# High parts one bank ahead of the low parts in the second product, and exchanged banks for half tiles

## The chip, the cores and the metric

The kernel runs on one core of a Trainium2 chip. The metric is the device time of one execution in microseconds. The unchanged kernel took 1166.94 us, the median of three runs (1163.73, 1166.94 and 1168.14).

## What is computed

Three stages over 7168 tokens of width 192, in float32:

- an attention-like convolution: for each token and each of 8 heads, a softmax over 7 taps weights the token and its 6 predecessors;
- a mixture of 8 experts in which each token goes to its best two, chosen by noisy logits;
- a second mixture of 8 experts in which each token goes to its best one.

An expert is two products with a ReLU between them. This is the part that matters here:

```python
h = np.maximum(x[mask] @ w1[e], 0.0)      # 192 -> 1024
out[mask] += top2_w[mask, k, None] * (h @ w2[e])   # 1024 -> 192
```

The second mixture is the same with one choice: `ye = h @ w2[e]`, times the gate's probability.

## The kernel before

**Numbers in two parts.** Matmuls run on fp32r operands, and each operand is split: a high part, which ScalarE rounds off, and a low part, which is the rest and which VectorE works out. The products high x high, high x low and low x high are added up in PSUM.

**Passes and tiles.** The first mixture is done in two passes (p = 0 and 1, one for each half of the tokens), the second in two more (p = 2 and 3). In each pass the tokens are sorted by expert into tiles of 256 rows (`T`); where at most 128 rows are left over for an expert, its last tile is a half tile of 128. Every engine has its own instruction stream and its own loop over the tiles, and they meet at semaphores. `g0 + j` is a tile's number over all passes.

**One full tile on TensorE** (`tile`, L1866): `up` (L1780) makes h, the product with w1, as 8 chunks `f` of 128 columns of w1 by 256 tokens, two chunks to each of the four banks of `ps_h` (banks 0 and 1 from chunks 0 to 3, banks 2 and 3 from chunks 4 to 7). Each chunk takes four matmuls (L1787, L1788, L1791, L1794); the first that needs xa_lo, the low part of the tile's rows, is L1791. Banks 0 and 1 are signalled after `up_low` (L1771), banks 2 and 3 at the end. Then `down` (L1839), the product with w2: for each of 8 chunks of h and each of the tile's two halves `u`, one matmul of the high part of h with both parts of w2 (L1849, 400 columns in the first two passes, 384 in the others) and one of the low part of h with the high part of w2 (L1850, 200 or 192 columns). Every fourth such matmul pair begins a bank, and there TensorE waits for the low part of that bank (L1843). After six pairs it turns the next tile's rows (`next_rows`, L1823): four transposes (L1764, L1765) of rows that GpSimd gathered by an indirect DMA (L584).

**ScalarE** (`tile`, L1476): `copy_high` (L1465) reads a bank of `ps_h` through the ReLU into `h_hi` (L1468), twice; then a middle part `mid_tile` (L1445) with side work and the next expert's w1a, after which it releases `ps_x`; then `copy_high` twice more; then the high parts of the next tile's rows (`split_rows`, L1395: xa_hi, L1397, and xb_hh, L1400, with the list for the next gather, L1504, between them); then it reads the low half of y (L1519 or L1525).

**VectorE** (`tile`, L1055): some side work (`before_splits`; in the first pass products of the convolution, L933), then four low parts `h_lo` (L1060), one a bank, each after that bank's `h_hi_ready`; then `after_splits` (sums of the convolution, L943), pieces of the next expert's weights (w1a L990, w1b L998), xa_lo and xb_lo of the next tile (L1042, L1043), w2 (L1013), and y of this tile (L1077 or L1080), which TensorE must have seen before its next `down`.

**A half tile.** `up_half` (L1803) makes h the other way round, 128 tokens by 512 columns, in banks 0 and 1 ("unturned rows"). ScalarE copies them out through the ReLU (`copy_rows`, L1471), TensorE turns them into banks 2 and 3 (L1819), and ScalarE reads those with `copy_high` into the second half of `h_hi`. The third read stands before ScalarE's middle part, the fourth behind it. VectorE runs all four low parts (L1060) in the order of the banks also here; the first two are of the unturned rows and nobody uses them. `down_half` (L1853) waits for the third low part before its first matmul (L1862) and for the fourth before its fifth pair; the next rows are turned after three pairs. `side` (L1746), work of TensorE for the routing of later passes, stands at the end of `up_half`.

## Time and profile before

| What | Value |
|---|---|
| Median of the runs | 1166.94 us (1163.73 to 1168.14) |
| The profiled execution's own time | 1160.52 us |
| Its span, first to last instruction | 1158.8 us |
| TensorE: matmuls busy | 1076.2 us, 93% |
| TensorE: weight loads busy | 1006.7 us, 87% |
| VectorE busy | 797.4 us, 69% |
| ScalarE busy | 561.2 us, 48% |
| GpSimd busy | 483.4 us, 42% |
| Mean granted TensorE clock | 0.977 |

The busy time of an engine is the sum over its instructions; matmuls are pipelined and their ends are modelled, so starts tell more than durations. In the rows further below an instruction is given by its start, its duration, its engine and line, what it writes and reads, and in brackets how long its engine stood idle before it and whose end released it.

### The profile page before, as it was taken

What the parts mean: (1) busy time and instruction counts of PE and PEld (TensorE: products, weight loads), DVE (VectorE), ACT (ScalarE), POOL (GpSimd) and SP (SyncE); (2) the same over time, 40 slices, a digit from 0 to 9 for tenths busy, and PEclk for the clock granted to TensorE, in tenths of its full rate; (3) what the DMA queues carried; (4) which work ended last, traced back from release to release, by engine and by line L of the source; (5) the groups of instructions that cost most, each with busy time, mean ns of one, the idle gap of its engine ahead of it and who ended that gap; (6) DMA issues with size and microseconds to landing.
All of it is one profiled execution on the core that took longest, in us unless ns stands there. A gap on an engine that the chain in (4) does not pass through costs nothing.

```text
span 1158.8 us, 29428 instructions
## 1 busy us (share of the span) xinstructions
PE 1076.2 (93%) x7894; PEld 1006.7 (87%) x7895; DVE 797.4 (69%) x1432; ACT 561.2 (48%) x1236; POOL 483.4 (42%) x527
## 2 busy tenths in 40 slices
PE   4998799889999999999999899999998898999995
PEld 3778699889999899999999899898988898898895
DVE  8998899998478655456656765556767765656652
ACT  3345335444634444455555344436665554555542
POOL 1000355555355444444444344444444543444442
PEclk9998899999999999999999999999999999999998
DMA  8449132342332233455544333337854643543510
GB/s 261 114 125 268 55 106 86 101 130 73 96 112 75 90 89 99 120 159 167 153 149 144 87 76 98 104 91 232 241 165 123 164 112 100 149 126 106 150 42 23
DMA packets 105109, 143.75 MB, mean 124 GB/s; under 512 B 27818, under 2 KB 82413, under 8 KB 104812
## 3 DMA queue, kind: packets, MB, share of 16 engines
q1 hardware_dynamic: 85612, 99.74, 29.8%
q0 software_dynamic: 19456, 43.53, 13.0%
q8 instruction: 17, 0.28, 0.1%
q14 instruction: 24, 0.20, 0.1%
HBM read 111.53 MB, written 35.09 MB: 127 GB/s over the span
## 4 chain that ended last, share of the span: by engine, by line
PE 75%; DVE 8%; DMA 6%; issue 6%; ACT 2%; DVEq 1%; POOL 1%; ACTq 0%; POOLq 0%; SPq 0%
PE ps_y L1849 20%; PE ps_y L1850 9%; PE ps_h L1787 7%; PE ps_h L1791 6%; PE ps_h L1788 6%; PE ps_h L1794 6%; DMA row<-x_rows,read_now 5%; PE ps_h L1775 4%; PE ps_h L1619 3%; PE ps_y L1862 2%; PE ps_x L1764 2%; PE ps_x L1765 2%; DVE h_lo L1060 2%; DMA w_more<-in_moe_w_dram 1%; PE ps_y L1863 1%
## 5 line engine op out<-in xcount | busy, mean ns | idle before, releaser
L1849 PE MATMUL ps_y<-w_hl,h_hi 128*128 128x400 f32 (+1 forms) x1344 | 411.5, 368 | 9.3 <-DVE h_lo L1060 7.6
L1060 DVE SCALAR_TENSOR_TENSOR h_lo<-ps_h,h_hi 128x512 fp32r<-128x512 f32 x404 | 259.4, 685 | 161.9 <-ACT h_hi L1468 129.0
L584 POOL DMA_INDIRECT row<-x_rows,read_now x200 | 225.3, 1127 | 303.9 <-ACT read_now L1504 259.1
L1850 PE MATMUL ps_y<-w_hl,h_lo 128*128 128x200 f32 (+1 forms) x1344 | 341.4, 254 | 0.0
L1468 ACT ACTIVATE h_hi<-ps_h 128x512 fp32r<-128x512 f32 x370 | 202.7, 595 | 222.7 <-PE ps_h L1775 137.7
L1849 PEld LDWEIGHTS ps_y<-w_hl,h_hi 128*128 128x128 f32 x1344 | 253.3, 189 | 13.2 <-DVE h_lo L1060 10.2
L1850 PEld LDWEIGHTS ps_y<-w_hl,h_lo 128*128 128x128 f32 x1344 | 257.5, 192 | 0.0
L1787 PE MATMUL ps_h<-xa_hi,w1a_hi 128*128 128x256 f32 x672 | 201.9, 300 | 3.1 <-ACT xa_hi L1397 2.5
L1791 PE MATMUL ps_h<-xa_lo,w1a_hi 128*128 128x256 f32 x672 | 190.5, 284 | 2.1 <-DVE xa_lo L1042 1.2
L1788 PE MATMUL ps_h<-xa_hi,w1a_lo 128*128 128x256 f32 x672 | 189.2, 282 | 0.0
L1794 PE MATMUL ps_h<-xb_hh,w1b_hl 128*128 128x256 f32 x672 | 188.6, 281 | 0.0
L602 POOL DMA_INDIRECT y_rows<-y,write_now x128 | 135.3, 1057 | 78.9 <-POOL write_now L597 58.5
L1787 PEld LDWEIGHTS ps_h<-xa_hi,w1a_hi 128*128 128x128 f32 x672 | 126.5, 188 | 15.8 <-ACT xa_hi L1397 3.0
L1791 PEld LDWEIGHTS ps_h<-xa_lo,w1a_hi 128*128 128x128 f32 x672 | 126.6, 188 | 3.1 <-DVE xa_lo L1042 1.8
L1788 PEld LDWEIGHTS ps_h<-xa_hi,w1a_lo 128*128 128x128 f32 x672 | 127.1, 189 | 0.0
L1794 PEld LDWEIGHTS ps_h<-xb_hh,w1b_hl 128*128 128x128 f32 x672 | 126.8, 189 | 0.0
L1397 ACT ACTIVATE xa_hi<-ps_x 128x256 fp32r<-128x256 f32 x101 | 38.8, 385 | 121.5 <-PE ps_x L1765 114.6
L602 POOL DMA_INDIRECT out_dram<-y,write_now x74 | 78.1, 1056 | 45.4 <-POOL write_now L597 33.2
L1042 DVE TENSOR_TENSOR xa_lo<-ps_x,xa_hi 128x256 fp32r<-128x256 f32 x101 | 42.4, 420 | 56.9 <-ACT xb_hh L1400 56.4
L1519 ACT ACTIVATE y_lo<-ps_y 128x400 f32<-128x400 f32 x64 | 32.3, 504 | 99.5 <-PE ps_y L1850 91.1
L597 POOL COPY write_now<-write_to 128x2 int32 x101 | 37.3, 369 | 103.1 <-DVE y L1077 52.0
L1077 DVE TENSOR_TENSOR y<-ps_y,y_lo 128x400 f32<-128x400 f32 x64 | 36.6, 572 | 46.0 <-ACT y_lo L1519 39.6
(245 smaller groups left out, 1665.1 us busy)
## 6 DMA issues: line engine op xcount, KB each, us to landing
w_raw<-in_moe_w_dram SPq DMA_DIRECT2D x32, 768.0 KB
w1a_raw<-in_moe_w_dram SPq DMA_DIRECT2D x32, 512.0 KB
w1b_raw<-in_moe_w_dram SPq DMA_DIRECT2D x64, 256.0 KB
x_rows<-tok SPq DMA_DIRECT2D x14, 512.0 KB, 3.3
x_rows<-tok SPq DMA_DIRECT2D x28, 256.0 KB
x_pad<-in_x_dram SPq DMA_DIRECT2D x2, 2688.0 KB, 11.7
row<-x_rows,read_now POOLq DMA_INDIRECT x200
x_pad<-y_rows SPq DMA_DIRECT2D x14, 200.0 KB
```

What stands on the lines that cost most here:

```text
L584: pool.indirect_dma_start(out=row[:, u, 0:XW if p < C else SCALED_W], out_offset=None, in_=x_rows[p], in_offset=bass.IndirectOffsetOnAxis( ...
L602: pool.indirect_dma_start(out=dst, out_offset=bass.IndirectOffsetOnAxis(ap=write_now[:, u:u + 1], axis=0), in_=y[:, u, 0:width], in_offset ...
L1042: nc.vector.tensor_tensor(xa_lo[:, :], ps_x[:, 0, :], xa_hi[:, :].bitcast(F32), ALU.subtract).then_inc(x_lo_ready, 1)
L1060: nc.vector.scalar_tensor_tensor(out=h_lo[:, i * GF:(i + 1) * GF, :], in0=ps_h[:, i, :].rearrange("p (f t) -> p f t", f=GF), scalar=0.0, i ...
L1468: act.activation(h_hi[:, i * GF:(i + 1) * GF, :], ps_h[:, i, :].rearrange("p (f t) -> p f t", f=GF), ACT.Relu).then_inc(h_hi_ready, 1)
L1775: last = nc.tensor.matmul(up_bank(f), w1b_hl[b][half, f * P:(f + 1) * P], xb_lo[half, :], start=(f // 2 == FC // 4), stop=(FC // 2 - 2 <= ...
L1787: nc.tensor.matmul(dst[f % 2], w1a_hi[b][:, cols], xa_hi[:, :], start=(f0 == 0), stop=False)
L1788: nc.tensor.matmul(dst[f % 2], w1a_lo[b][:, cols], xa_hi[:, :], start=False, stop=False)
L1791: nc.tensor.matmul(dst[f % 2], w1a_hi[b][:, cols], xa_lo[:, :], start=False, stop=False)
L1794: last = nc.tensor.matmul(dst[f % 2], w1b_hl[b][:, cols], xb_hh[:, :], start=False, stop=(f >= FC - 2))
L1849: nc.tensor.matmul(first, h_hi[:, i, cols], both_w, start=(i == 0), stop=False)
L1850: last = nc.tensor.matmul(second, h_lo[:, i, cols], high_w, start=False, stop=(i == FC - 1))
```

## The change

In full tiles, `down` runs over five steps k. Step k does the four high matmuls of bank k (k below 4) and, alternating with them, the four low matmuls of bank k - 1 (k above 0). High matmuls wait for `h_hi_ready`, low ones for `h_lo_ready`. The next rows are turned at the start of step 2.

In half tiles, the unturned rows are made in banks 2 and 3 and turned into banks 0 and 1, and the turned parts go to the first half of `h_hi`. ScalarE's copies of unturned rows have a semaphore of their own, `rows_copied`; the second turned bank signals three banks at once, so that VectorE's low parts of banks 2 and 3 (of rows that nobody uses) come last. `down_half` has three steps in the manner of `down`. `side` and the turning of the next rows stand after its first four high matmuls.

Since VectorE may still be reading banks 2 and 3 when the product is over, `up` waits for all of the tile before's low parts ahead of its fifth chunk, and `up_half` ahead of its first.

```diff
--- before.py
+++ after.py
@@ -249,7 +249,7 @@
         y_loaded = [sem(f"y_loaded{c}") for c in range(C)]
         scales_copied = sem("scales_copied")
         scales_seen = sem("scales_seen")
-        rows_seen = sem("rows_seen")
+        rows_copied = sem("rows_copied")
         w1a_loaded = sem("w1a_loaded")
         w1b_loaded = sem("w1b_loaded")
         w2_loaded = sem("w2_loaded")
@@ -1184,6 +1184,7 @@
             for p in (1, 2):
                 dve.sem_inc(columns_done[p + 1], FIRST[p])
             dve.sem_inc(y_ready, 1)
+            dve.sem_inc(h_lo_ready, NG)
             nc.vector.memset(h_hi[:, :, :].bitcast(F32), 0.0).then_inc(zeros_made, 1)
             for w in gate_w_b:
                 nc.vector.memset(w[0:DR, 1, :], 0.0).then_inc(consts_made, 1)
@@ -1471,7 +1472,13 @@
             def copy_rows(g0, j, i):
 
                 act.wait_ge(h_ps, (g0 + j) * NG + (i + 1))
-                act.activation(h_rows[i], ps_h[:, i, :], ACT.Relu).then_inc(h_hi_ready, 1)
+                act.activation(h_rows[i], ps_h[:, NG // 2 + i, :], ACT.Relu).then_inc(rows_copied, 1)
+
+            def copy_turned(g0, j, i, signals=1):
+
+                act.wait_ge(h_ps, (g0 + j) * NG + (NG // 2 + i + 1))
+                act.activation(h_hi[:, i * GF:(i + 1) * GF, :], ps_h[:, i, :].rearrange("p (f t) -> p f t", f=GF),
+                               ACT.Copy).then_inc(h_hi_ready, signals)
 
             def tile(p, g0, n, b0, full, j, e, ahead):
 
@@ -1483,11 +1490,14 @@
                 with act.Else():
                     for i in range(NG // 2):
                         copy_rows(g0, j, i)
-                    copy_high(g0, j, NG // 2)
+                    copy_turned(g0, j, 0)
                 mid_tile(p, j, b0, ahead)
                 with act.If(j < full):
-                    copy_high(g0, j, NG // 2)
-                copy_high(g0, j, NG // 2 + 1)
+                    for i in range(NG // 2, NG):
+                        copy_high(g0, j, i)
+                    act.sem_inc(rows_copied, 2)
+                with act.Else():
+                    copy_turned(g0, j, 1, 1 + NG // 2)
                 if ahead is not None:
                     with act.If(j == b0):
                         split_w1b(*ahead)
@@ -1777,9 +1787,15 @@
                     if f == FC // 2 - 1:
                         last.then_inc(h_ps, 2)
 
+            def lows(g, k):
+
+                return (g + 1) * NG + k
+
             def up(p, g0, j, b):
 
                 for f0 in range(0, FC, 2):
+                    if f0 == FC // 2:
+                        pe.wait_ge(h_lo_ready, lows(g0 + j, 0))
                     pair = (f0, f0 + 1)
                     dst = [up_bank(f) for f in pair]
                     for f in pair:
@@ -1803,7 +1819,9 @@
             def up_half(p, g0, j, b):
 
                 for i in range(NG // 2):
-                    dst = ps_h[:, i, :]
+                    dst = ps_h[:, NG // 2 + i, :]
+                    if i == 0:
+                        pe.wait_ge(h_lo_ready, lows(g0 + j, 0))
                     cols = slice(i * 512, (i + 1) * 512)
                     nc.tensor.matmul(dst, xa_hi[:, 0:P], w1a_hi[b][:, cols], start=True, stop=False)
                     nc.tensor.matmul(dst, xa_hi[:, 0:P], w1a_lo[b][:, cols], start=False, stop=False)
@@ -1814,11 +1832,10 @@
                     pe.wait_ge(x_lo_ready, 2 * (g0 + j) + 2)
                     nc.tensor.matmul(dst, xb_lo[:, 0:P], w1b_hl[b][:, cols], start=False, stop=True).then_inc(h_ps, 1)
                 for i in range(NG // 2):
-                    pe.wait_ge(h_hi_ready, (g0 + j) * NG + (i + 1))
+                    pe.wait_ge(rows_copied, (g0 + j) * 2 + (i + 1))
                     for q in range(FC // 2):
-                        last = nc.tensor.transpose(ps_h[:, NG // 2 + i, q * P:(q + 1) * P], h_rows[i][:, q * P:(q + 1) * P], ident[:, :])
+                        last = nc.tensor.transpose(ps_h[:, i, q * P:(q + 1) * P], h_rows[i][:, q * P:(q + 1) * P], ident[:, :])
                     last.then_inc(h_ps, 1)
-                side(p, j)
 
             def next_rows(p, g0, n, j):
 
@@ -1838,29 +1855,52 @@
 
             def down(p, g0, n, b, j):
 
-                for i, f in enumerate(sorted(range(FC), key=place_of)):
-                    if i % GF == 0:
-                        pe.wait_ge(h_lo_ready, (g0 + j) * NG + (i // GF + 1))
-                    if i == FC // 4 + 1:
+                order = sorted(range(FC), key=place_of)
+                for k in range(NG + 1):
+                    if k == 2:
                         next_rows(p, g0, n, j)
-                    for u in range(SUB):
+                    if k < NG:
+                        pe.wait_ge(h_hi_ready, (g0 + j) * NG + (k + 1))
+                    for m in range(GF * SUB):
+                        u = m % SUB
                         cols = slice(u * P, (u + 1) * P)
-                        first, second, both_w, high_w = down_operands(p, b, f, u)
-                        nc.tensor.matmul(first, h_hi[:, i, cols], both_w, start=(i == 0), stop=False)
-                        last = nc.tensor.matmul(second, h_lo[:, i, cols], high_w, start=False, stop=(i == FC - 1))
+                        if k < NG:
+                            i = k * GF + m // SUB
+                            first, _, both_w, _ = down_operands(p, b, order[i], u)
+                            nc.tensor.matmul(first, h_hi[:, i, cols], both_w, start=(i == 0), stop=False)
+                        if k > 0:
+                            i = (k - 1) * GF + m // SUB
+                            if m == 0:
+                                pe.wait_ge(h_lo_ready, lows(g0 + j, k))
+                            _, second, _, high_w = down_operands(p, b, order[i], u)
+                            last = nc.tensor.matmul(second, h_lo[:, i, cols], high_w, start=False, stop=(i == FC - 1))
                 last.then_inc(y_ps, 1)
 
+            def half_at(f):
+                return f // 2
+
+            def half_cols(f):
+                return slice(f % 2 * P, f % 2 * P + P)
+
             def down_half(p, g0, n, b, j):
 
-                for f in range(FC):
-                    if f % 4 == 0:
-                        pe.wait_ge(h_lo_ready, (g0 + j) * NG + (NG // 2 + f // 4 + 1))
-                    if f == FC // 2 - 1:
+                for k in range(3):
+                    if k == 1:
+                        side(p, j)
                         next_rows(p, g0, n, j)
-                    at, cols = FC // 2 + f // 2, slice(f % 2 * P, f % 2 * P + P)
-                    first, second, both_w, high_w = down_operands(p, b, f, 0)
-                    nc.tensor.matmul(first, h_hi[:, at, cols], both_w, start=(f == 0), stop=False)
-                    last = nc.tensor.matmul(second, h_lo[:, at, cols], high_w, start=False, stop=(f == FC - 1))
+                    if k < 2:
+                        pe.wait_ge(h_hi_ready, (g0 + j) * NG + (k + 1))
+                    for m in range(FC // 2):
+                        if k < 2:
+                            f = k * (FC // 2) + m
+                            first, _, both_w, _ = down_operands(p, b, f, 0)
+                            nc.tensor.matmul(first, h_hi[:, half_at(f), half_cols(f)], both_w, start=(f == 0), stop=False)
+                        if k > 0:
+                            f = (k - 1) * (FC // 2) + m
+                            if m == 0:
+                                pe.wait_ge(h_lo_ready, lows(g0 + j, k))
+                            _, second, _, high_w = down_operands(p, b, f, 0)
+                            last = nc.tensor.matmul(second, h_lo[:, half_at(f), half_cols(f)], high_w, start=False, stop=(f == FC - 1))
                 last.then_inc(y_ps, 1)
 
             def tile(p, g0, n, s, b, j, rows):
```

## Rows read from the trace of the kernel before

**Rows 1.** The page, chain that ended last, shares of the span by engine.
```profile
PE 75%; DVE 8%; DMA 6%; issue 6%; ACT 2%; DVEq 1%; POOL 1%; ACTq 0%; POOLq 0%; SPq 0%
```

**Rows 2.** Groups by line: count, busy us, mean ns, idle us before them and releasers.
```profile
L1849 PE MATMUL ps_y<-w_hl,h_hi 128*128 128x400 f32 (+1 forms) x1344 | 411.5, 368 | 9.3 <-DVE h_lo L1060 7.6 <-issue 1.7
...
L1850 PEld LDWEIGHTS ps_y<-w_hl,h_lo 128*128 128x128 f32 x1344 | 257.5, 192 | 0.0
...
L1862 PE MATMUL ps_y<-w_hl,h_hi 128*128 128x400 f32 (+1 forms) x136 | 50.0, 418 | 18.7 <-DVE h_lo L1060 18.0 <-issue 0.7
```

**Rows 3.** Timeline of a plain half tile: start us, us, engine, what, idle before.
```profile
1048.25 0.59 ACT L1468 ACTIVATE h_hi<-ps_h 128x512 fp32r<-128x512 f32 x1
1049.10 0.60 ACT L1468 ACTIVATE h_hi<-ps_h 128x512 fp32r<-128x512 f32 x1 [0.26 <-issue]
...
1048.39 2.04 DVE L1060 SCALAR_TENSOR_TENSOR h_lo<-ps_h,h_hi 128x512 fp32r<-128x512 f32 x3 [0.48 <-ACT tok_T_b L1474]
1052.26 0.42 DVE L1042 TENSOR_TENSOR xa_lo<-ps_x,xa_hi 128x256 fp32r<-128x256 f32 x1 [1.83 <-ACT xb_hh L1400]
...
1048.41 0.66 PE L1819 MATMUL ps_h<-ident,tok_T_b 128*128 128x128 f32 x4 [0.25 <-ACT tok_T_b L1474]
1049.73 0.44 PE L1862 MATMUL ps_y<-w_hl,h_hi 128*128 128x384 f32 x1 [0.67 <-DVE h_lo L1060]
...
1052.78 0.34 PE L1791 MATMUL ps_h<-xa_lo,w1a_hi 128*128 128x256 f32 x1
```

**Rows 4.** Timeline of three half tiles in which VectorE is late.
```profile
655.59 2.47 DVE L1060 SCALAR_TENSOR_TENSOR h_lo<-ps_h,h_hi 128x512 fp32r<-128x512 f32 x4
...
657.53 0.45 PE L1862 MATMUL ps_y<-w_hl,h_hi 128*128 128x400 f32 x1 [2.39 <-DVE h_lo L1060]
...
662.23 0.28 PE L1791 MATMUL ps_h<-xa_lo,w1a_hi 128*128 128x256 f32 x1
...
865.93 2.48 DVE L1060 SCALAR_TENSOR_TENSOR h_lo<-ps_h,h_hi 128x512 fp32r<-128x512 f32 x4
...
870.94 0.33 PE L1791 MATMUL ps_h<-xa_lo,w1a_hi 128*128 128x256 f32 x1
...
895.60 2.47 DVE L1060 SCALAR_TENSOR_TENSOR h_lo<-ps_h,h_hi 128x512 fp32r<-128x512 f32 x4
...
902.14 0.28 PE L1791 MATMUL ps_h<-xa_lo,w1a_hi 128*128 128x256 f32 x1
```

**Rows 5.** Windows: length, busy of PE, PEld, DVE, ACT, POOL, then granted clock, DMA.
```profile
659.10:662.00 2.90, 2.90 (x13) 2.88 (x13) 1.37 (x6) 0.86 (x3) 1.19 (x2) 0.51 0.58 126
```

**Rows 6.** Timeline of a half tile of the first pass.
```profile
212.57 2.47 DVE L1060 SCALAR_TENSOR_TENSOR h_lo<-ps_h,h_hi 128x512 fp32r<-128x512 f32 x4
214.97 1.34 DVE L943 TENSOR_TENSOR prod<-prod 128x1152 f32<-128x1152 f32 x1
...
212.98 0.60 ACT L1468 ACTIVATE h_hi<-ps_h 128x512 fp32r<-128x512 f32 x1 [0.59 <-ACT taps L1345]
...
219.22 0.28 PE L1791 MATMUL ps_h<-xa_lo,w1a_hi 128*128 128x256 f32 x1
```

**Rows 7.** Timeline of a half tile with w1b behind the low parts.
```profile
1107.05 2.03 DVE L1060 SCALAR_TENSOR_TENSOR h_lo<-ps_h,h_hi 128x512 fp32r<-128x512 f32 x3 [0.48 <-ACT tok_T_b L1474]
1109.11 1.39 DVE L998 TENSOR_TENSOR w1b_hl<-w1b_raw,w1b_hl 64x512 f32 x2
...
1111.44 0.34 PE L1791 MATMUL ps_h<-xa_lo,w1a_hi 128*128 128x256 f32 x1
```

**Rows 8.** Timeline, TensorE: a wait for gathered rows.
```profile
807.15 0.33 PE L1764 MATMUL ps_x<-ident,row 128*128 128x128 f32 x1 [1.94 <-DMA row<-x_rows,read_now]
```

**Rows 9.** Timeline, TensorE: the wait ahead of the product in a full tile.
```profile
355.80 0.45 PE L1849 MATMUL ps_y<-w_hl,h_hi 128*128 128x400 f32 x1 [0.86 <-DVE h_lo L1060]
```

**Rows 10.** Timeline, TensorE: two pairs in a row in a full tile.
```profile
708.24 0.37 PE L1849 MATMUL ps_y<-w_hl,h_hi 128*128 128x400 f32 x1
...
708.54 0.36 PE L1849 MATMUL ps_y<-w_hl,h_hi 128*128 128x400 f32 x1
```

## The prediction

> **What bounds the kernel now.** I read the chain of waits first: TensorE holds 75% of the chain that ended last [rows 1]. So a part of the change is worth what it takes from TensorE's idle time, and nothing elsewhere. The groups by line then tell how many tiles there are of each sort: the high-part matmul of a half tile stands 136 times, 8 to a tile, so 17 half tiles; L1849 stands 1344 times, 16 to a tile, so 84 full ones. The same lines show in their idle time what can be won: 18.0 us ahead of the second product of half tiles, 7.6 us ahead of that of full tiles, both behind VectorE's low parts (L1060) [rows 2]. Last the timeline, for the order inside a tile.
>
> A plain half tile [rows 3]: ScalarE reads the second bank of unturned rows, then the first turned bank (1048.25, done 1048.84), then the second (1049.10, done 1049.70). VectorE has begun low parts of the unturned rows, which nobody uses; the first useful one is its third, so TensorE's product begins only at 1049.73, and L1791 of the next tile at 1052.78.
>
> **Removed: the wait for low parts before a half tile's product.** The product can begin when ScalarE is done with the first turned bank, at 1048.90 instead of 1049.73: 0.8 us. After four high matmuls (0.7 us) and the next rows' four transposes (0.44 us) both parts of the banks are there. The eight pairs still cost their 0.29 us each, so the tile's matmuls end 0.8 us earlier. But what is late next is VectorE: the two low parts that nobody uses now stand behind the useful ones. They wait for the second turned bank (1049.70), so three operations of about 0.62 us (four in 2.47 us [rows 4]) end at 1051.6, where all were done at 1050.4. xa_lo of the next tile (0.42 us) is then ready at 1052.1, and L1791 waits for it, some 0.3 us. L1791 moves from 1052.78 to 1052.1: 0.65 us. Five tiles are like this (I take 0.6 each) and the last of all has no next tile (0.8): **3.7 us**.
>
> **Where VectorE comes late.** In five half tiles VectorE was busy when the turned rows were there and then ran its four operations in one piece, the useless ones first. In the one at 655.59 [rows 4] TensorE stood 2.39 us, and after that its granted clock was 0.51 (1.2 GHz) from 659.10 to 662.00 [rows 5]; L1791 of the next tile came at 662.23. Now the product starts when the first turned bank is read, about 655.0, low parts are ready at 656.3 and 656.9, before they are needed; matmuls end about 657.95, the piece of four ends at 658.06 as before, xa_lo at 658.5. Gain 3.7. By the same working, the piece of 895.60 ends at 898.07, xa_lo at 898.5, against L1791 at 902.14: 3.6. The piece of 865.93 is cut by the wait for the second turned bank (one operation, then three from 867.2), ends at 869.1, xa_lo at 869.6, against 870.94: 1.3. In the first pass [rows 6] the side work (now inside the product, some 1.2 us) and ScalarE's reading of it come ahead of the second turned bank, which is done near 214.2 instead of 213.58; VectorE's three remaining low parts end at 216.2, the sums at L943 (1.34 us) at 217.6, xa_lo at 218.1, against L1791 at 219.22: 1.1, and a second such tile the same. Sum 3.7 + 3.6 + 1.3 + 1.1 + 1.1 = **10.8 us**. Nearly half of it is the slow clock that the long waits left behind.
>
> **Where the change costs.** In four half tiles VectorE has the next expert's w1b to split behind its low parts [rows 7]: low parts to 1109.1, 1.39 us of splitting, xa_lo, L1791 at 1111.44. With the useless ones last, the low parts end at 1110.35, the split at 1111.74, xa_lo at 1112.1: 0.7 us lost. Two of the four are followed by a wait for gathered rows (the longer one 1.94 us [rows 8]) that swallows it, as the gather's list comes no later than before; the other two cost **1.4 us**. Of the last two half tiles, one has list matmuls as a cover already, one waits for rows anyway: nothing.
>
> **Full tiles.** The first product matmul now needs the high part alone, and a low part is first needed 0.9 us later (four high matmuls and one more). The wait at 355.80 [rows 9] (0.86 us) goes whole. At four of the other waits VectorE's y of the tile before, which TensorE must have too, is the next to end, 0.5 us before the low part; three of these stand in one stretch in which VectorE is busy throughout. I take 0.5 and 0.2, and 0.3 for that stretch: **1.9 us** of the 7.6. The next rows are turned after 8 high and 4 low matmuls, not 6 and 6: 0.1 us later, which is covered: 8 high and 12 low matmuls still stand behind them, where five pairs are enough in the half tile of [rows 3] for xa_lo to come without a wait worth a row. Nor are the added semaphore counts on ScalarE (one a full tile) on the path: ScalarE is busy 48%.
>
> **The order of matmuls.** A pair starts 0.30 us after the pair before (708.24 and 708.54 [rows 10]), though 600 columns at 2.4 GHz are 0.25 us; I read it as the load of the next weights showing behind the short low matmul. Each low matmul is still followed by one load, so I take nothing. Bounds: four low matmuls now follow each other. If each of the last three hid its load, it is the pair's excess less, 0.04 us: 3 x 84 x 0.04 = 10 us at most; if a load showed whole (0.19 us [rows 2]) instead of some 0.11, 3 x 84 x 0.08 = 20 us more. The Trainium skill (TensorE: Matmul & The Clock Gate, Back-to-back issue gap) gives for a warm isolated stream the columns at 2.4 GHz and 2.5 ns: 86 ns for a low matmul of 200 columns. By that rule the three would be 21 ns shorter than I take, an estimate of 5 us for the kernel; the trace of before has no two low matmuls in a row.
>
> **New waits for rows.** In half tiles the next rows are wanted 1.0 us earlier. In 12 of them they came early enough for the old place; how early isn't seen. Between 0 and 12 us are given back; nearer 0, since most waits of TensorE for rows stand in tiles where the weights are loaded too. I take 2.
>
> **Sum**: 3.7 + 10.8 - 1.4 + 1.9 - 2 = 13 us. The profiled execution took 1160.5 us (span 1158.8, 1.7 around it), so 1147.5; it is 6.4 us under the median of the runs shown, 1166.9, and against that the forecast is 1154.
>
> **Rivals.** *Rows and low parts take the wait's place.* Half tiles get so short that gather and VectorE's later low parts set their length. For it: xa_lo is late in my own working by 0.3 us and more, and rows have stopped TensorE for 1.94 us. Against it: the three largest gains come from tiles whose low parts end where they did. Price: the 3.7 and 1.9 go, and 2 of the 10.8 with them; gain 5 to 6, 1161.
>
> *Slower: the block of low matmuls shows its loads.* Its place is the end of each of 84 full products, its price 20 us as above; less the 13, that is 7 slower, 1174. It decides from 0.05 us a low matmul (13 over 252). Against it: transposes of 128 columns follow each other at 0.11 us to 0.13 us (four of them in 0.66 us, the last one's drain included [rows 3]), loads and all.
>
> *The lows come cheaper.* The estimate by the rule above: 1149.
>
> *It doesn't do what it says.* The early high parts could stay unused, since ps_x is free only once ScalarE is through its middle part, and y and the split weights must be there too; then only the plain tiles win: 13 - 9 = 4, 1163.
>
> **Numbers.** Forecast 0.52, rows and low parts 0.20, slower 0.08, cheaper lows 0.10, not what it says 0.10. A measurement can tell about 0.5% here, 5.8 us, so faster is below 1161.1. Faster: 0.52 + 0.10 + half of 0.20 = 0.72; same 0.20; slower 0.08. The range takes in the cheaper lows and the rows, 1145 to 1164.
>
> **What would show it.** TensorE's wait for L1060 ahead of half tiles falls from 18 us to under 2 and no clock of 0.5 stands behind it; L1791's wait for xa_lo rises by some 6 us; the waits for rows rise by 2; in the four tiles with w1b behind, L1791 comes 0.7 us later after the tile's start. Wrong it would be if four low matmuls at the end took over 0.13 us each, or if TensorE's waits for rows rose by over 6 us.

## The result, and the profile after

| What | Before | Changed |
|---|---|---|
| Median of the runs (8 each) | 1165.53 us (1160.42 to 1170.09) | 1149.20 us (1143.19 to 1159.31) |
| The profiled execution's own time | 1160.52 us | 1148.81 us |
| Its span | 1158.8 us | 1147.1 us |
| Mean granted TensorE clock | 0.977 | 0.978 |

The ratio is 0.9857 with an interval of 0.9818 to 0.9897: 16 us less, where 13 were forecast, and the 1149.2 us lie inside the range of 1145 to 1164.

The chain that ended last, shares of the span by engine, answers to [rows 1]:

```profile
PE 76%; DMA 8%; DVE 6%; issue 5%; ACT 2%; POOL 1%; DVEq 1%; ACTq 1%; POOLq 0%; SPq 0%; another core or an unknown queue 0%
```

VectorE's share of the chain fell from 8% to 6%, and DMA's rose from 6% to 8%: already here one sees what was removed and what stands next in line.

The groups by line of the changed kernel, as in [rows 2] (L1870 and L1876 are the high and the low matmuls of full tiles, L1897 the high ones of half tiles):

```profile
L1870 PE MATMUL ps_y<-w_hl,h_hi 128*128 128x400 f32 (+1 forms) x1344 | 370.6, 360 | 2.2 <-DVE y L1080 0.8 <-ACT h_hi L1469 0.8 <-issue 0.5
...
L1876 PE MATMUL ps_y<-w_hl,h_lo 128*128 128x200 f32 (+1 forms) x1344 | 293.6, 259 | 1.3 <-DVE h_lo L1060 1.3
...
L1774 PE MATMUL ps_x<-ident,row 128*128 128x128 f32 x202 | 50.6, 277 | 15.8 <-DMA row<-x_rows,read_now 11.8 <-ACTq L1464 2.0 <-DMA row<-x_rows,read_from 1.5
...
L1897 PE MATMUL ps_y<-w_hl,h_hi 128*128 128x400 f32 (+1 forms) x136 | 39.7, 380 | 2.2 <-ACT h_hi L1480 1.6 <-DVE y L1080 0.6
```

The idle time ahead of the second product was 18.7 us in half tiles and 9.3 in full ones; it is 2.2 and 3.5. That makes 22 us less, and the time fell by 16. The waits of TensorE show part of the difference (us in total, times, longest):

```profile
PE ps_x L1774 <- DMA row<-x_rows,read_now: 11.8, 10, 2.2
...
PE ps_h L1803 <- DVE w1b_hl L998: 3.8, 3, 1.4
...
PE ps_h L1807 <- DVE xa_lo L1042: 2.5, 5, 1.0
...
PE ps_x L1774 <- ACTq L1464: 2.0, 2, 1.0
```

Rows were 9.0 us in 8 waits before, xa_lo 1.2 in 3. The waits for w1b and for ScalarE (ACTq) are new.

**The late half tile of [rows 4].** The same tile after, timeline:

```profile
652.04 0.57 DVE L1077 TENSOR_TENSOR y<-ps_y,y_lo 128x400 f32<-128x400 f32 x1
...
652.52 2.47 DVE L1060 SCALAR_TENSOR_TENSOR h_lo<-ps_h,h_hi 128x512 fp32r<-128x512 f32 x4
652.84 1.00 PE L1897 MATMUL ps_y<-w_hl,h_hi 128*128 128x400 f32 x4 [0.90 <-ACT h_hi L1480]
654.02 0.43 PE L1897 MATMUL ps_y<-w_hl,h_hi 128*128 128x400 f32 x1
654.29 0.26 PE L1903 MATMUL ps_y<-w_hl,h_lo 128*128 128x200 f32 x1
```

VectorE's piece of four takes 2.47 us as before. TensorE's wait fell from 2.39 to 0.90 us: the product starts beside the piece instead of behind most of it. The row names ScalarE's h_hi, the last to end before it; but that is the second turned bank (652.64), which the first four matmuls don't need. What they did need, beside the first bank, is y of the tile before, and it ended at 652.61. And in the stretch behind, where [rows 5] had a granted clock of 0.51, the windows of the changed kernel show full clock (the sixth value after the length, the counts in brackets aside):

```profile
655.00:662.00 7.00, 6.89 (x56) 6.42 (x55) 4.92 (x15) 2.71 (x6) 4.30 (x5) 1.00 0.57 141
```

**The plain half tile of [rows 3].** The same tile after, TensorE, VectorE and ScalarE:

```profile
1037.64 0.59 ACT L1480 ACTIVATE h_hi<-ps_h 128x512 fp32r<-128x512 f32 x1
...
1038.26 0.69 DVE L1060 SCALAR_TENSOR_TENSOR h_lo<-ps_h,h_hi 128x512 fp32r<-128x512 f32 x1 [1.62 <-ACT h_hi L1480]
1038.28 0.97 PE L1897 MATMUL ps_y<-w_hl,h_hi 128*128 128x384 f32 x4
...
1039.18 1.89 DVE L1060 SCALAR_TENSOR_TENSOR h_lo<-ps_h,h_hi 128x512 fp32r<-128x512 f32 x3 [0.23 <-issue]
...
1040.57 0.70 PE L1903 MATMUL ps_y<-w_hl,h_lo 128*128 128x192 f32 x5
...
1040.98 0.41 DVE L1042 TENSOR_TENSOR xa_lo<-ps_x,xa_hi 128x256 fp32r<-128x256 f32 x1
...
1041.32 0.38 PE L1803 MATMUL ps_h<-xa_hi,w1a_hi 128*128 128x256 f32 x1
...
1041.66 0.28 PE L1807 MATMUL ps_h<-xa_lo,w1a_hi 128*128 128x256 f32 x1
```

The product follows the turning with no wait, and VectorE's three remaining low parts end at 1041.07, xa_lo right behind them, just in time.

**The order of matmuls.** Five low matmuls at a full tile's end, after:

```profile
706.37 0.37 PE L1870 MATMUL ps_y<-w_hl,h_hi 128*128 128x400 f32 x1
706.58 0.70 PE L1876 MATMUL ps_y<-w_hl,h_lo 128*128 128x200 f32 x5
707.12 0.30 PE L1803 MATMUL ps_h<-xa_hi,w1a_hi 128*128 128x256 f32 x1
```

A single low matmul takes some 0.26 us, its drain included, so the five follow each other at (0.70 - 0.26) / 4 = 0.11 us, the value that the prediction took. The Trainium skill (TensorE: Matmul & The Clock Gate, Back-to-back issue gap) has a formula for an isolated matmul's gap, by which one of 200 columns would take an estimated 86 ns; at a granted clock of 1.00 this trace does not show it. The same section says that in a stream of loads and matmuls both set the spacing. That fits this trace, where each low matmul has a load of its own (191 ns long on average), but no run shows by itself that the loads set the 0.11 us. A full tile without waits took, from 403 us on in the first mixture, 9.83 us before and 9.81 after, in the median.

### The profile page after: what moved, and what is told of

Its sections match the earlier page's. It is cut to its first block, busy times and chain, and to the rows that moved or that the text cites. A ratio compares the mean times of both kernels' runs of the same rounds, so it can differ in the third digit from the quotient of the medians.

```text
span 1147.1 us, 29950 instructions
## 1 busy us (share of the span) xinstructions
PE 1076.0 (94%) x7894; PEld 1004.6 (88%) x7895; DVE 794.6 (69%) x1432; ACT 561.0 (49%) x1236; POOL 485.9 (42%) x527
## 4 chain that ended last, share of the span: by engine, by line
PE 76%; DMA 8%; DVE 6%; issue 5%; ACT 2%; POOL 1%; DVEq 1%; ACTq 1%; POOLq 0%; SPq 0%; another core or an unknown queue 0%
PE ps_y L1870 19%; PE ps_y L1876 10%; PE ps_h L1803 8%; PE ps_h L1807 6%; DMA row<-x_rows,read_now 6%; PE ps_h L1810 6%; PE ps_h L1804 6%; PE ps_h L1785 4%; PE ps_h L1629 3%; PE ps_x L1774 2%; PE ps_x L1775 2%; PE ps_y L1897 1%; DMA w_more<-in_moe_w_dram 1%; DVE prod L703 1%; PE ps_y L1903 1%
## 5 line engine op out<-in xcount | busy, mean ns | idle before, releaser
L1060 DVE SCALAR_TENSOR_TENSOR h_lo<-ps_h,h_hi 128x512 fp32r<-128x512 f32 x404 | 258.4, 684 | 179.5 <-ACT h_hi L1469 119.5
L1870 PE MATMUL ps_y<-w_hl,h_hi 128*128 128x400 f32 (+1 forms) x1344 | 370.6, 360 | 2.2 <-DVE y L1080 0.8
L584 POOL DMA_INDIRECT row<-x_rows,read_now x200 | 228.5, 1142 | 284.9 <-ACT read_now L1514 233.8
L1469 ACT ACTIVATE h_hi<-ps_h 128x512 fp32r<-128x512 f32 x336 | 182.5, 596 | 231.8 <-PE ps_h L1785 137.2
L1876 PE MATMUL ps_y<-w_hl,h_lo 128*128 128x200 f32 (+1 forms) x1344 | 293.6, 259 | 1.3 <-DVE h_lo L1060 1.3
L1870 PEld LDWEIGHTS ps_y<-w_hl,h_hi 128*128 128x128 f32 x1344 | 244.5, 188 | 3.4 <-ACT h_hi L1469 2.5
L1876 PEld LDWEIGHTS ps_y<-w_hl,h_lo 128*128 128x128 f32 x1344 | 235.6, 191 | 2.3 <-DVE h_lo L1060 2.3
L1774 PE MATMUL ps_x<-ident,row 128*128 128x128 f32 x202 | 50.6, 277 | 15.8 <-DMA row<-x_rows,read_now 11.8
```

The lines of the kernel that those rows point to most:

```text
L584: pool.indirect_dma_start(out=row[:, u, 0:XW if p < C else SCALED_W], out_offset=None, in_=x_rows[p], in_offset=bass.IndirectOffsetOnAxis( ...
L1060: nc.vector.scalar_tensor_tensor(out=h_lo[:, i * GF:(i + 1) * GF, :], in0=ps_h[:, i, :].rearrange("p (f t) -> p f t", f=GF), scalar=0.0, i ...
L1469: act.activation(h_hi[:, i * GF:(i + 1) * GF, :], ps_h[:, i, :].rearrange("p (f t) -> p f t", f=GF), ACT.Relu).then_inc(h_hi_ready, 1)
L1774: nc.tensor.transpose(ps_x[:, 0, u * P:(u + 1) * P], row[:, u, 0:P], ident[:, :])
L1870: nc.tensor.matmul(first, h_hi[:, i, cols], both_w, start=(i == 0), stop=False)
L1876: last = nc.tensor.matmul(second, h_lo[:, i, cols], high_w, start=False, stop=(i == FC - 1))
```

## Experiments

Each was timed in five rounds beside the kernel before on the same chip. The intervals are 0.5 to 0.8% wide, 6 to 9 us, so the traces tell more than the times about a single tile. "Tile" is the time from one tile's first matmul with xa_lo to the next one's, as L1791 in the prediction. E1 to E4, E5 to E8 and E9 to E12 ran on one chip each.

| Run | Half tiles | Ratio to before, interval |
|---|---|---|
| E1 changed | exchange and lead | 0.9871 (0.9833 to 0.9908) |
| E2 | as before | 0.9963 (0.9940 to 0.9987) |
| E3, full tiles as before | exchange and lead | 0.9922 (0.9892 to 0.9951) |
| E4, E8 unused rows' low parts left out | exchange and lead | 0.9824 (0.9789 to 0.9860), 0.9842 (0.9802 to 0.9882) |
| E5 list first | exchange and lead | 0.9902 (0.9865 to 0.9940) |
| E6 side work back | exchange and lead | 0.9829 (0.9789 to 0.9869) |
| E7 | exchange alone, side work in the new place | 0.9995 (0.9962 to 1.0027) |
| E9 w2 behind y | exchange and lead | 0.9832 (0.9804 to 0.9860) |
| E10, with E6 | exchange alone, side work in the old place | 0.9891 (0.9852 to 0.9930) |
| E11 | lead alone, side work in the old place | 0.9835 (0.9796 to 0.9874) |
| E12, E4 + E6 + E9 | exchange and lead | 0.9778 (0.9741 to 0.9815) |

"Exchange" is the use of the last two banks for unturned rows, with the useful low parts first; "lead" is that high parts start ahead of low ones.

**E1: the changed kernel once more**, as the ground for the others.

> The changed kernel once more, beside the parts of it. Both theories: about 16 us faster than the kernel before (1.4%).

Median 1147.94 us against 1163.60 of the kernel before, 16 us less, as in the first comparison.

**E2 and E3: the two halves of the change.** E2 leaves ScalarE's half-tile part, `up_half` and `down_half` as they were and keeps the new `down`; E3 the other way round. The edit of E2's half-tile wait:

```diff
-                        pe.wait_ge(h_lo_ready, (g0 + j) * NG + (NG // 2 + f // 4 + 1))
+                        pe.wait_ge(h_lo_ready, lows(g0 + j, NG // 2 + f // 4 + 1))
```

> Only the full tiles are changed (high parts one bank ahead); half tiles are as before. Theory (the gain sits in the half tiles): 3 to 5 us faster than before; TensorE's waits for low parts ahead of half tiles stay at 18 us. Rival (the order of matmuls in the 84 full tiles brings it): 10 us or more.

> Only the half tiles are changed (banks exchanged, high parts ahead); full tiles are as before. Theory: 10 to 12 us faster than before, and the waits for low parts in full tiles stay near 7.6 us. Rival (the full tiles bring it): 5 us or less.

E2 took 1159.53 us, 4 less than before; E3 1155.60, 8 less (9 by the ratio). Each trace keeps the wait whose part was left alone. E2:

```profile
PE ps_y L1884 <- DVE h_lo L1060: 19.5, 15, 3.1
```

E3:

```profile
PE ps_y L1866 <- DVE h_lo L1060: 8.7, 13, 2.2
```

By the ratios the parts give 0.4% and 0.8%, together 1.2%, against 1.3% in E1: they add up within their intervals. By them half tiles carry two thirds of the gain, and full tiles more than the 1.9 us of the sum. The tiles say the same more sharply: the 25 full tiles among the first 33 that do not stand right behind a half tile took 268.7 us together before and 269.4 in E3, and 263.1 to 264.0 in each of the twelve profiled runs that have the lead in full tiles.

**E4 and E8: leave out the low parts nobody uses.** VectorE skips the low parts of banks 2 and 3 in half tiles; the outputs don't depend on them. E8 also has E5's edit.

```diff
+                for i in range(NG // 2):
+                    low_part(i)
+                with dve.If(dve.snap(half_at) == j):
+                    dve.wait_ge(h_lo_ready, (g0 + j + 1) * NG + NG // 2)
+                    dve.sem_inc(h_lo_ready, NG // 2)
+                with dve.Else():
+                    for i in range(NG // 2, NG):
+                        low_part(i)
```

> The changed kernel, but VectorE leaves out the two low parts of a half tile that nobody uses. Theory (they stand ahead of the w1b split and of xa_lo and cost about 0.8 us in each of four half tiles): TensorE's waits for w1b_hl (3.8 us) and xa_lo (2.5 us) fall to about 1 us together, time 2 to 4 us below the changed kernel. Rival (gathered rows are late anyway, or the added branch costs as much): the waits go but time stays within 1 us, with the waits for rows up by 2 us or more.

> Unused low parts left out and the list copied first, both together. Theory (each takes away what holds up the other): 6 to 9 us below the changed kernel, about 1142 where before is 1165. Rival: the sum of the two alone or less.

In the cut of the edit above, `low_part` is one round of the loop that was there. E4 took 1145.42 us, 2.5 below E1, which the intervals do not tell apart; E8 took 1149.08, 8 below E5 of the same chip. But the waits aimed at hardly fell: w1b from 4.8 to 3.6 us, xa_lo from 3.4 to 2.7. The timeline of VectorE in a half tile with w1b behind tells why:

```profile
1097.37 0.69 DVE L1063 SCALAR_TENSOR_TENSOR h_lo<-ps_h,h_hi 128x512 fp32r<-128x512 f32 x1 [0.23 <-ACT h_hi L1493]
1099.05 1.38 DVE L998 TENSOR_TENSOR w1b_hl<-w1b_raw,w1b_hl 64x512 f32 x2 [0.98 <-DVEq L1071]
```

Two operations of about 0.62 us are gone, but 0.98 us of nothing stand in their place, spent in VectorE's own queue at the branch and its waits. Three of these four tiles shrank from 7.9 to 7.7 us and the fourth from 9.5 to 8.8, none by the 1.2 us of the two operations.

**E5: the gather's list ahead of xa_hi.**

```diff
-                act.activation(xa_hi[:, :], ps_x[:, 0, :], ACT.Copy).then_inc(x_hi_ready, 1)
                 if between is not None:
                     between()
+                act.activation(xa_hi[:, :], ps_x[:, 0, :], ACT.Copy).then_inc(x_hi_ready, 1)
```

> The changed kernel, but ScalarE copies the list of the next gather (and the scales) ahead of xa_hi, so that the gather is issued 0.4 to 0.6 us earlier in every tile. Theory (in plain half tiles rows are late because the gather is issued late, the rest is a fixed latency): the waits for rows fall from 11.8 us to 6 to 8, time 3 to 5 us below the changed kernel. Rival (the queues are full of weight loads and set the arrival): waits for rows stay within 2 us, time the same or up to 1 us longer since xa_hi comes later.

It took 1157.40 us, 4 us worse than E1 by the ratios (the intervals overlap), and waits for rows rose from 12.0 to 16.6 us. No reasoning in the expectations had this. Take the full tile at 524 us (525 in E1). The copy of the list (L1514) ends 7.64 us into the tile in both: ScalarE's branches around it take some 0.4 us, and xa_hi used to run beside them. What did move is xb_hh, 0.27 us later; with it VectorE's split of w2 (at 9.02 instead of 8.75), the end of the second gather (11.62 instead of 11.35) and TensorE's first matmul on those rows (15.22 instead of 14.98). That tie between w2 and the gather led to E9.

**E6: the side work back at the end of `up_half`.**

```diff
                     if k == 1:
-                        side(p, j)
                         next_rows(p, g0, n, j)
```

> The changed kernel, but a half tile's side work stands at the end of the first product again. Theory: in the two half tiles of the first pass the wait for ps_x (0.99 us each) goes and the time falls by 1 to 2 us; elsewhere nothing. Rival (VectorE's sums set the end of those two tiles): the wait goes, time within 0.5 us.

Both first-pass half tiles went from 10.57 and 10.56 to 9.87 us each, and the wait for ScalarE (`ACTq L1464`, 0.99 us each) is gone. The time, 1148.57 us beside a before of 1166.11, is not told from the changed kernel's; for the two tiles the gain is shown, for the kernel it is not.

**E7: high parts wait for low ones again, in the exchanged banks.**

```diff
                     if k < 2:
                         pe.wait_ge(h_hi_ready, (g0 + j) * NG + (k + 1))
+                        pe.wait_ge(h_lo_ready, lows(g0 + j, k + 1))
```

> The changed kernel, but a half tile's product waits for the low part of each bank as before; the exchanged banks stay. It tells the exchange from the high parts' lead. Theory (in the five tiles where VectorE is late, the exchange brings the most, since the useful low parts come first; in the plain ones rows hold TensorE anyway): 2 to 4 us slower than the changed kernel. Rival (the lead of the high parts is what counts): 8 us or more slower.

1167.26 us, no gain left at all, where 2 to 4 us more than the changed kernel were expected: the rival was right. The price is not spread evenly: the two first-pass half tiles cost 5.5 us each. Timeline of TensorE in the first:

```profile
216.96 1.70 PE L1898 MATMUL ps_y<-w_hl,h_hi 128*128 128x400 f32 x4 [2.94 <-DVE h_lo L1060]
218.46 0.47 PE L1687 MATMUL ps_route<-gate_w_b,taps 128*128 128x32 f32 x2
...
221.47 0.47 PE L1774 MATMUL ps_x<-ident,row 128*128 128x128 f32 x1 [0.99 <-ACTq L1464]
...
223.09 0.70 PE L1898 MATMUL ps_y<-w_hl,h_hi 128*128 128x400 f32 x1 [0.51 <-DVE h_lo L1060]
```

And the window behind the wait:

```profile
217.00:223.50 6.50, 4.99 (x18) 4.18 (x19) 1.15 (x2) 1.90 (x6) 1.21 (x2) 0.50 0.25 86
```

TensorE stands for 2.94 us, then the side work, which in the old order would have filled that wait, comes behind it, at half clock (0.50, 1.2 GHz). So the change's place for `side` costs 0.7 us a tile with the lead (E6) and 5.0 us without it (16.08 us beside the 11.03 of E10).

**E10: E7 with the side work back (exchange alone).**

> Banks exchanged, side work at the end of the first product, each bank of a half tile's product waiting for its low part: the exchange without the lead of the high parts. Theory, after the run with low waits and moved side work came out no faster than before: what was lost there is lost in the two half tiles of the first pass, where wait and side work now followed each other; so with the side work back, 6 to 10 us faster than before. Rival (the lead is what counts everywhere): within 3 us of before's time less the 4 us of the full tiles, 1159 to 1162.

1155.58 us, 12 less than its before, more than the 6 to 10 expected, and 0.7% less than E2, which has neither in half tiles. The first-pass half tiles took 11.03 and 11.04 us, the plain ones 7.0 to 8.1.

**E11: the old banks and order of low parts, high parts ahead (lead alone).** From the kernel of E2, with `down_half` in the steps of the change but on the second half of `h_hi`, and `side` at the end of `up_half`:

```diff
-                        pe.wait_ge(h_hi_ready, (g0 + j) * NG + (k + 1))
+                        pe.wait_ge(h_hi_ready, (g0 + j) * NG + (NG // 2 + k + 1))
...
-                                pe.wait_ge(h_lo_ready, lows(g0 + j, k))
+                                pe.wait_ge(h_lo_ready, lows(g0 + j, NG // 2 + k))
```

> High parts ahead in full and half tiles, but a half tile's rows and turned parts in the banks of before, so that VectorE works out the two unused low parts first. Theory (where VectorE is late, the useful low parts must come first): the five late half tiles keep most of their wait, now ahead of the first low matmul; 5 to 8 us faster than before, 8 or more slower than the changed kernel. The four tiles with w1b behind the low parts lose nothing. Rival: as fast as the changed kernel.

1146.56 us, 0.9835: as fast as with the exchange. The fair neighbour is E6 (0.9829), since both have the side work in its old place. This is the run that my theory of the half tiles did not survive: the five late half tiles with the tiles behind them took 108.0 us before, 95.4 here, 95.1 in E6 and 98.7 in E10. Its half tile with w1b behind, VectorE and TensorE:

```profile
1092.74 2.04 DVE L1060 SCALAR_TENSOR_TENSOR h_lo<-ps_h,h_hi 128x512 fp32r<-128x512 f32 x3 [0.48 <-ACT tok_T_b L1475]
...
1093.24 0.96 PE L1886 MATMUL ps_y<-w_hl,h_hi 128*128 128x384 f32 x4
...
1094.05 0.27 PE L1765 MATMUL ps_x<-ident,row 128*128 128x128 f32 x1
...
1094.40 0.42 PE L1886 MATMUL ps_y<-w_hl,h_hi 128*128 128x384 f32 x1
...
1094.66 0.25 PE L1892 MATMUL ps_y<-w_hl,h_lo 128*128 128x192 f32 x1
...
1094.80 1.39 DVE L998 TENSOR_TENSOR w1b_hl<-w1b_raw,w1b_hl 64x512 f32 x2
```

The third low part in VectorE's order, the first useful one, is done some 1.3 us after 1092.74, about 1094.1; TensorE needs it at 1094.66. Four high matmuls, four transposes and one more high matmul cover the two useless low parts, and no wait stands there. The same tile of the changed kernel, VectorE and then TensorE:

```profile
1096.59 1.89 DVE L1060 SCALAR_TENSOR_TENSOR h_lo<-ps_h,h_hi 128x512 fp32r<-128x512 f32 x3 [0.23 <-ACT h_hi L1480]
1098.51 1.39 DVE L998 TENSOR_TENSOR w1b_hl<-w1b_raw,w1b_hl 64x512 f32 x2
...
1100.04 0.38 PE L1803 MATMUL ps_h<-xa_hi,w1a_hi 128*128 128x256 f32 x1 [1.37 <-DVE w1b_hl L998]
```

There the split of w1b is later and TensorE waits 1.37 us for it. Three of the four tiles of this kind take 6.6 to 6.8 us in E11 and 7.9 in E1, the fourth 8.4 and 9.5. The first-pass ones take 9.7 to 9.8 us against 10.6, but that is the place of the side work (9.9 in E6). Against that E11 loses 0.3 to 0.4 us in three half tiles where VectorE is late.

**E9: w2 split behind y.** To test whether VectorE's split of w2 (L1013) holds the gather that runs beside it:

```diff
                 before_results(j)
-                if weights:
-                    split_w2_ahead(p, j)
...
                     last.then_inc(y_ready, 1)
+                if weights:
+                    split_w2_ahead(p, j)
```

> The changed kernel, but VectorE splits the next expert's w2 (L1013, two operands in SBUF, 1.75 us) after y instead of before it. Theory (the second gather of a tile is held on GpSimd until that split ends: 1.54 us instead of 1.0, 2.71 where the split begins with it): in tiles with a w2 split the second gather takes 1.0 us, the waits for rows fall from 12 us to 8 or less, time 3 to 8 us below the changed kernel. Rival (rows are late for the traffic of weights, whatever GpSimd does): gathers shorten, waits for rows stay within 2 us, time within 1 us.

The waits for rows fell from 12.0 us to 2.8, and other waits stand beside them:

```profile
PE ps_y L1876 <- DVE h_lo L1060: 3.4, 4, 1.3
...
PE ps_x L1774 <- DMA row<-x_rows,read_now: 2.8, 4, 1.4
...
PE ps_y L1870 <- DVE w_hl L1013: 1.9, 2, 1.4
PE ps_y L1870 <- ACT h_hi L1469: 1.9, 3, 0.8
```

But the span, 1145.0 us, stayed (E1: 1145.2). Three of the plain half tiles are 0.4 to 1.1 us shorter, and the tile behind each is 0.4 to 1.3 us longer, since w2, high parts and low parts are late there. The wait for rows was a real one, and behind it VectorE and ScalarE were nearly as late. The median, 0.9832, is not told from E1's.

**E12: E4, E6 and E9 together.**

> The changed kernel with all three: unused low parts left out, side work at the end of the first product, w2 split after y. Theory: 5 to 10 us below the changed kernel, 1138 to 1143 where before is 1165. Rival (what one gives the others take as a wait): within 2 us of the best of them alone, 1145.

1141.53 us beside a before of 1167.90: ratio 0.9778, the lowest median of all, and below the changed kernel's 0.9871 with intervals apart; from E4, E6, E9 and E11 the intervals do not tell it. In its trace the waits for rows are nearly gone, and no wait of the same size took their place; TensorE's waits with their causes:

```profile
PE ps_h L1820 <- DVE xa_lo L1045: 3.5, 6, 1.0
PE ps_y L1890 <- DVE h_lo L1063: 2.6, 5, 0.9
PE ps_y L1884 <- ACT h_hi L1482: 2.5, 4, 0.8
PE ps_h L1816 <- DVE w1b_hl L998: 2.4, 3, 1.1
...
PE ps_x L1787 <- DMA row<-x_rows,read_now: 0.8, 2, 0.6
```

E11 with E9 was not tried, and would be the next.

## Why the prediction was right, and where it was not

The traces of before and after, set beside each other tile by tile from the first matmul with xa_lo (127.2 and 133.0 us) to the end, differ by 17.5 us. The stretch ahead of it was 5.8 us longer in the changed kernel's profiled execution, so the spans differ by only 11.7. That stretch is work whose code the change doesn't touch. It ended between 127.2 and 136.2 us in the fourteen profiled executions, which had mean granted clocks from 0.91 down to 0.84 in their first 130 us. The kernel before was profiled only once, so whether the change has a part in it stays open.

| Term | Forecast | Trace |
|---|---|---|
| Five late half tiles, with the tiles behind | +10.8 | +11.1 |
| Plain half tiles and the last | +3.7, -2 for rows | +1.2 |
| Four half tiles with w1b | -1.4 | -3.4, and +3.7 in the tiles behind |
| Full tiles of the first pass | +1.9 for all full tiles | +5.4 |
| One full tile at 968 | 0 | -1.4, with slow clock, which E1 does not repeat |
| All other tiles | 0 | +0.9 |
| Order of matmuls | 0 | 0.04 a tile at most |

- **The late tiles** carried the result, and the mechanism held in the main: the long waits are gone, and so is the slow clock behind them in all but one. Before, it stood behind four of the five. In the second first-pass tile of the profiled execution it still stood after the change, 0.51 from 262.0 to 264.5 us, behind the new wait of 0.99 us for ScalarE; E1 has none there, and the tile took 10.60 and 10.56 us. E11 shows that the lead alone takes these waits away. Single sizes were off. The tiles at 652 and 892 gave 3.06 and 2.96 us where 3.7 and 3.6 were forecast: behind L1060 the next to be late was y of the tile before (0.90 us above, 0.60 us in the other). The second first-pass tile gave 2.45 us instead of 1.1, since its wait before (2.81 us) was followed by slow clock (0.67 from 262 to 268 us) that the step on that tile did not count. The side work inside the product cost 0.7 us in each of the two first-pass tiles, as E6 shows.
- **Plain half tiles** were forecast too high. (Five times 0.6 and 0.8 are 3.8, not 3.7.) The step worked out 0.65 us a tile with xa_lo as the next to be late. That holds for one, the tile of [rows 3] (0.51 us, and 0.33 in the tile behind). In the four others it was rows: new waits of 0.69 to 1.25 us. The "2 us for rows" was set by the hope that most row waits stand elsewhere; in these tiles they took 2.5 of the 3.7 us. Waits for rows rose by 2.8 us in total, xa_lo's by only 1.3 where 6 were named.
- **The tiles with w1b** lost 0.71 to 1.09 us each, where 0.7 was worked out. The step let two of the four be swallowed by rows; in fact three of them gave it back in the next tile. Behind 978 a wait for rows of 1.50 us was gone; behind 791 the wait stayed (2.12 us, before 1.94) and the tile was still 1.58 us shorter, with slow clock before (granted 0.50 from 808.7 us) and none after; behind 926 it was a full tile's wait for low parts (0.62 us). Of these only the last is the change's own work; the others differ between runs of one kernel too.
- **Full tiles** were forecast too low, and this is the largest error in the sum. The wait at 355.80 went whole, and the first tile's wait fell from 2.17 to 1.26 us. But the other gains are spread over tiles that the step left out: eight more gave 0.27 to 0.65 us each. They had waits ahead of the product of up to 0.54 us, which the profile puts down to VectorE or to "issue" and which the sum had mostly left out, and the product itself took 5.12 us there before and 4.99 after, from its first matmul to its last. E2 measured some 4 us for the whole part, twice the 1.9.
- **What the sum was right about for the wrong reason**: it credited the plain tiles and the late ones to the exchange of banks together with the lead. E11 shows that the lead alone does it, E10 beside E2 that the exchange alone gives about half (0.7% of the 1.3% that both give in E6), and E6 beside E11 that together they give no more than the lead. The two cover the same wait; for the lead no run shows a cost, while the exchange costs 1.2 us in three of the four tiles with w1b behind and 1.1 in the fourth.
- **The total** is nearer than its terms, and that is partly luck. In the traces the terms add up to 17.5 us, of which the 3.7 behind the tiles with w1b and the -1.4 are mostly the chance of two executions; full tiles gave 3.5 us more than forecast. The share of the slow clock is large: from the first tile to the last one TensorE had a granted clock of 0.50 for 20.5 us before and for 6.8 after (3.4 in E1). If half of such a time is lost, an estimate, that is 6.8 of the 17.5 us.
- **Rivals.** Rows did take the wait's place in four of the plain tiles, so that rival was right there, but not in the late tiles nor in the full ones, whose gain it wrote off. That the early high parts stay unused is excluded by the late tiles: with the lead in E6 they and the tiles behind them take 3.6 us less than without it in E10. The slower case (loads showing, over 0.13 us a low matmul) is excluded by the 0.11 us measured, and so are cheaper lows (0.086).

Open: E5 is slower than the changed kernel by its median and its row waits, but the size (4 us against E1 by the ratios, 9 against E6) is not settled; its profiled execution also had the slow clock for 20.5 us, E1's for 3.4. Nor is it shown which of its three parts gives E12 its advantage; each alone is inside the others' intervals.

## What to carry to other kernels

When a product of high and low parts waits for the low ones, issue the high matmuls first; the matmuls you then have in hand may cover so much that no reordering of the late engine's work is needed, and such a reordering pushes useful work behind useless. Count separately the waits that a slow clock follows: five of 101 tiles, with the tiles behind them, gave 11 of the 17.5 us here. And do not leave out small waits because each is short: ten full tiles gave 0.3 to 0.9 us each, which is half as much again. Try each half of a two-part change alone, since two parts may cover the same wait, and moving side work into a new place may cost more without the other part (E7).

## What the runs showed of the hardware

**A gather on GpSimd is held by a VectorE operation beside it.** GpSimd in the changed kernel, two gathers of one tile:

```profile
791.86 1.14 POOL L584 DMA_INDIRECT row<-x_rows,read_now  x1 [1.17 <-issue]
793.30 2.71 POOL L584 DMA_INDIRECT row<-x_rows,read_now  x1 [0.30 <-issue]
```

and VectorE in the same stretch:

```profile
793.08 0.41 DVE L1043 TENSOR_TENSOR xb_lo<-ps_x,xb_hh 128x256 fp32r<-128x256 f32 x1
793.41 1.74 DVE L1013 TENSOR_TENSOR w_hl<-w_raw,w_hl 128x1536 f32 x1
```

The second gather takes 2.71 us instead of 1.0 and ends at 796.01, 0.86 us after L1013 (795.15). In this trace all 20 gathers of over 1.3 us that L1013 runs beside end 0.83 to 0.86 us after it; the long gathers and scatters beside L990 and L943, also with both inputs in SBUF, do the same (0.82 to 0.88). Gathers and scatters that overlap L1013 but had begun 0.15 us or more before it took 0.97 to 1.17 us, all but the one at 901.94 below. The 100 that began during an L1060, which reads one input from PSUM, took 0.98 to 1.02 us. The longest, at 901.94, took 4.50 us beside four VectorE operations in a row, L1013 the last. E9 moved L1013 and with it the number of gathers and scatters over 1.3 us, from 50 to 33, and the waits for rows, from 12.0 to 2.8 us. The Trainium skill (SBUF — State Buffer, Who interferes with whom) says that a Vector operation with two SBUF inputs contends with GpSimd operations that read SBUF, not with those that only write it, and infers that `tensor_tensor` does not stall a DMA, whose descriptors need the write interface. The measurement decides: here a TENSOR_TENSOR with both inputs in SBUF held an indirect gather. The gather reads its list of rows, `read_now`, from SBUF, so the first statement may be the reason; no run tells that read from the writing of descriptors.

**A wait can cost more than itself.** The tile at 791 took 11.59 us with a row wait of 1.66 us in E1, and 14.11 us (at 792) with one of 2.60 us in E6: 0.94 us more of waiting, 2.52 us more of tile. The window behind the longer wait in E6:

```profile
801.30:804.50 3.20, 3.20 (x17) 3.20 (x17) 0.76 (x2) 2.27 (x5) 0.99 (x1) 0.65 0.83 317
```

The mean granted clock is 0.65 there, a mix of 1.2 and 2.4 GHz. The length of the wait does not settle it alone: in the first trace of the changed kernel the same wait was 2.12 us, no slow clock followed, and the tile took 12.06 us, 0.47 more than in E1 for 0.46 more of waiting. Such waits, with a slow clock behind them in one execution and none in another, may be why runs of one kernel scatter by 1%. The eight executions of the changed kernel fit that (span 1141.4 us at a mean granted clock of 0.983, 1157.5 at 0.971), but no run was made to test it.
